# A sequence-mixing kernel on one core: the rows of a chunk are put in another order by the band, and the output goes out in runs of 8, 7 and 3 tokens

## What is computed

```python
# x: (8, 4224, 192), weight: (8 heads, 7 taps); all float32 in DRAM
w = softmax(weight)                                  # per head, over the 7 taps
y[b, s, h, :] = sum_k w[h, k] * x[b, s - 6 + k, h, :]   # causal convolution; 24 columns a head
W_tok = ((y @ w_q) @ (y @ w_k).T) / 8                # d_hyper = 64
out = relu(W_tok @ y) @ w_out                        # (8, 4224, 192)
```

## Time and profile before

| | |
|---|---|
| median of 3 runs | 185.6 us (184.69 to 186.93) |
| the profiled execution: its time, its span | 185.72 us, 184.0 us |
| DMA queue q0 (loads of x): packets, MB | 36,832, 13.96 |
| DMA queue q1 (stores, weights): packets, MB | 14,448, 26.45 |
| mean granted clock of TensorE | 0.952 of full speed |

### The profile page before, as it was taken

The page is one execution under the profiler, slowest core; times in us unless marked ns, Lnnn a source line. Parts: engine busy times, 40 slices in busy tenths (PEclk is TensorE's granted clock), DMA queues, the critical chain, the costliest instruction groups (busy, mean ns, idle before and its releaser), DMA issues.

```text
span 184.0 us, 5172 instructions
## 1 busy us (share of the span) xinstructions
PE 154.7 (84%) x2213; PEld 102.9 (56%) x2213; DVE 126.4 (69%) x207; ACT 124.5 (68%) x257; POOL 28.4 (15%) x35
## 2 busy tenths in 40 slices
PE   6876989999999999999599999892999898993500
PEld 2335745744867865667466776572755665572300
DVE  5346589786878886999668983991669979662100
ACT  2222479999686988968499759834479799894300
POOL 7910039952310600000000000000000000000000
PEclk9997899999999999999999999999699999999665
DMA  3999949999999999999999991890589699888896
GB/s 33 154 196 197 199 57 120 192 193 193 192 296 332 211 194 212 338 276 297 249 277 338 204 223 61 236 302 6 155 259 316 229 303 269 248 281 284 251 287 193
DMA packets 51302, 40.72 MB, mean 221 GB/s; under 512 B 38928, under 2 KB 44560, under 8 KB 51280
## 3 DMA queue, kind: packets, MB, share of 16 engines
q0 software_dynamic: 36832, 13.96, 64.1%
q1 hardware_dynamic: 14448, 26.45, 45.6%
HBM read 28.39 MB, written 25.95 MB: 295 GB/s over the span
## 4 chain that ended last, share of the span: by engine, by line
DMA 41%; PE 29%; ACT 10%; SPq 8%; DVE 3%; issue 2%; DVEq 0%; ACTq 0%; POOLq 0%
DMA xw<-in_x_dram 30%; PE ps L322 9%; DMA out_dram<-out_sb 8%; PE ps L923 7%; PE ps L940 6%; ACT out_sb L318 5%; SPq L978 5%; DMA wqf<-in_moe_w_q_dram 3%; PE ps L877 2%; ACT y L318 2%; PE ps L865 2%; PE ps L772 1%; SPq L969 1%; PE ps L323 1%; PE ps L690 1%
## 5 line engine op out<-in xcount | busy, mean ns | idle before, releaser
L318 ACT COPY out_sb<-ps 128x768 f32<-128x768 f32 (+2 forms) x68 | 38.9, 611 | 17.0 <-PE ps L940 10.9
L318 ACT CAST y<-ps 128x432 bf16<-128x432 f32 (+3 forms) x60 | 36.5, 650 | 12.7 <-PE ps L322 9.7
L671 DVE STREAM_TRANSPOSE yt<-y 128x864 uint32<-128x864 uint32 x32 | 33.4, 1059 | 4.6 <-ACT y L318 4.6
L895 ACT ACTIVATE rt<-ps 128x512 bf16<-128x512 f32 (+4 forms) x65 | 33.5, 559 | 2.8 <-PE ps L865 2.2
L896 DVE TENSOR_SCALAR rt<-ps 128x512 bf16<-128x512 f32 (+4 forms) x47 | 29.4, 651 | 8.1 <-PE ps L865 3.9
L500 POOL DMA_DIRECT2D xw<-in_x_dram x30 | 28.0, 948 | 34.7 <-DVE xw L511 16.4
L318 DVE COPY out_sb<-ps 128x384 f32<-128x384 f32 (+2 forms) x34 | 22.5, 684 | 15.5 <-PE ps L940 10.4
L322 PE MATMUL ps<-y 120*128 120x192 bf16 (+1 forms) x288 | 30.4, 253 | 2.7 <-ACT y L318 2.7
L940 PE MATMUL ps<-wol,rt 128*128 128x192 bf16 (+3 forms) x280 | 30.1, 258 | 0.2
L923 PE MATMUL ps<-woh,rt 64*128 64x192 bf16 (+1 forms) x280 | 26.1, 261 | 3.9 <-DVE out_sb L318 2.9
L322 PEld LDWEIGHTS ps<-y 120*128 120x128 bf16 (+1 forms) x288 | 24.7, 101 | 7.9 <-ACT y L318 3.2
(11 more groups left out here) (88 smaller groups left out, 119.5 us busy)
## 6 DMA issues: line engine op xcount, KB each, us to landing
out_dram<-out_sb SPq DMA_DIRECT2D x42, 384.0 KB, 5.5
xw<-in_x_dram POOLq DMA_DIRECT2D x7, 864.0 KB, 27.5
xw<-in_x_dram POOLq DMA_DIRECT2D x7, 672.0 KB, 30.6
out_dram<-out_sb SPq DMA_DIRECT2D x14, 288.0 KB, 5.2
out_dram<-out_sb SPq DMA_DIRECT2D x24, 96.0 KB, 3.4
out_dram<-out_sb SPq DMA_DIRECT2D x12, 192.0 KB, 2.8
xw<-in_x_dram POOLq DMA_DIRECT2D x7, 168.0 KB, 17.7
xw<-in_x_dram POOLq DMA_DIRECT2D x2, 432.0 KB, 8.2
```

What stands on the lines that cost most here:

```text
L318: return e.copy(dst, src) if op.engine == "ACT" else e.tensor_copy(dst, src)
L671: return e.transpose(YT[:, tb, ks, :].rearrange("p c d -> p (c d)"), Y[:, yb, ks, :].rearrange("p c d -> p (c d)").bitcast(U32))
L895: return e.activation(dst, src, AF.Relu)
```

## The change

Column j of the band makes row j of a chunk, so the order of the band's columns decides which token a partition holds. After the change, row 32a + 4m + i of a long chunk holds token 15m + 4a + i (m = 0 to 7; for a = 3, i = 3 the column is zero). Behind the transposes and `fin`, a partition of the output then has 15 tokens in a row for 16 chunks: 8 of them in the stretch of blocks 0 and 1, 7 in that of blocks 2 and 3. Each stretch is one DMA of 128 runs of 6,144 or 5,376 bytes. For the short chunks a second band, `BAND2`, puts token 3s + a on row 32a + s; the tail is one DMA of 128 runs of 2,304 bytes. With it:

- `BAND2` is built by two more PE operations (`spread2`) and two evacuations; the convolution of a group with short chunks takes two matmuls a head in place of one (14 chunks with `BAND`, 4 with `BAND2`);
- the short chunks load all 128 rows, so `zero_x`, `zero_xl` and the wait of the loads for them are gone; batch 1's first chunk is loaded in two pieces like batch 0's, so its `zero_c` is gone;
- block 3 is 32 columns wide in the queries, `mix` and `relu` (before 24); `fin` leaves out the zero fourth token of block 3; the tail's queries are evacuated in order, not strided;
- in the last batch only stretches 0 and 2 go out in halves, each half one DMA;
- `PLAN` is another: its convolution, evacuation and store entries stand in another order, with 107 joined evacuations (91 before). Seven store entries now stand together behind batch 3 (`586S 467S 477S 596S 544S 558S 572S`); four stood together there before (`581S 462S 539S 472S`). It ends `... 992A2 997A2 1022D 1021D 1023S 994S 999S`.

```diff
-    CW, RW, BL = 120, 96, 32
+    CW, RW, BL, RUN = 120, 96, 32, 15
-    zero_x = zero(XW[RW:128, 0, NM:, :], "zero_x")
+    zero_o = zero(OWN[:, RUN:16], "zero_o")
-    zero_xl = zero_later(XW[RW:128, 1:, NM:, :], "zero_xl")
+    zero_b = zero_later(BAND2[:, :, RW:], "zero_b")
...
-                    bank(op.bank)[:, 64 * q : 64 * q + 64].rearrange("p (i h) -> p i h", h=4),
-                    STEPT[0:112, 112 - 16 * q : 240 - 16 * q],
-                    TAPS[0:112, :, 4 * half : 4 * half + 4],
+                    bank(op.bank).rearrange("p (a m i h) -> p m a i h", a=NB, m=8, i=4)[:, q],
+                    STEPT[0:112, 112 - RUN * q : 240 - RUN * q],
+                    TAPS[0:112, :, 4 * half : 4 * half + 4].rearrange("p (a i) h -> p a i h", a=NB),
...
+        def spread2(e, op, half=half):
+            last = None
+            for q in range(7):
+                n = min(5, BL - 5 * q)
+                last = halves(
+                    e,
+                    bank(op.bank)[:, 0 : 4 * RW].rearrange("p (a s h) -> p a s h", a=3, h=4)[:, :, 5 * q : 5 * q + n, :],
+                    STEPT[0:112, 112 - RUN * q : 240 - RUN * q],
+                    TAPS[0:112, 0 : 3 * n, 4 * half : 4 * half + 4].rearrange("p (u a) h -> p a u h", a=3),
...
-                parts.append(rows(NM, NR, 0, ROWS, RW))
+                parts.append(rows(NM, NR, 0, 128, RW))
...
-                needs=([zero_xl if b else zero_x] if cs and cs[-1] == NCC - 1 and dst.shape[0] == ROWS and b < NX else []) + free,
+                needs=free,
...
+        runs = [(BAND, c0, sum(c < NM for c in cs)), (BAND2, max(c0, NM), sum(c >= NM for c in cs))]
...
+                    for band, c, m in runs:
+                        last = halves(
+                            e,
+                            PS[:, o + (c - c0) * GRP : o + (c - c0 + m) * GRP],
+                            band[:, h, :],
+                            XW[:, xb, c : c + m, GRP * h : GRP * h + GRP],
...
-        ns = (2 * TW, TW) if tail else [16 * TOKENS[a] for a in BLOCK[j]]
+        ns = (2 * TW, TW) if tail else (NQ, NQ)
...
-        pieces = 2 if b == B - 1 and not tail else 1
+        pieces = 2 if b == B - 1 and j % 2 == 0 and not tail else 1
...
-            todo = [(i, a) for i in (q, q + 1) for a in range(2) if not tail or (i, a) != (1, 1)]
+            todo = [(i, a) for i in (q, q + 1) for a in range(2) if i < has[a]]
...
                     if tail:
-                        for k in range(3):
-                            dst = bass.AP(out_t, (b * S + t0[NM] + BL * k) * D, [[D, BL], [RW * D, NR], [1, D]])
-                            sent.append((e.dma_start(dst, OUT[:, oslot, k % 2, k // 2, :]), 16))
-                        return sent
-                    for z in range(2):
-                        src = OUT[0 : rows[z], oslot, z, qa:qz, :].rearrange("p q d -> p (q d)")
-                        dst = bass.AP(
-                            out_t,
-                            (b * S + t0[16 * (j // 2)] + BL * BLOCK[j][z] + qa) * D,
-                            [[CW * D, 16], [nt * D, rows[z] // 16], [1, (qz - qa) * D]],
-                        )
-                        sent.append((e.dma_start(dst, src), 16))
-                    return sent
+                        dst = bass.AP(out_t, (b * S + t0[NM]) * D, [[3 * D, 128], [1, 3 * D]])
+                        return e.dma_start(dst, OUT[:, oslot, 0, 0:3, :].rearrange("p q d -> p (q d)"))
+                    t = b * S + t0[16 * (j // 2)] + 8 * (j % 2) + qa
+                    if pieces > 1:
+                        dst = bass.AP(out_t, t * D, [[RUN * D, 128], [4 * D, 2], [1, (qz - qa) * D]])
+                        return e.dma_start(dst, OUT[:, oslot, :, qa:qz, :].rearrange("p a q d -> p a (q d)"))
+                    m = sum(has) * D
+                    src = OUT[:, oslot, :, :, :].rearrange("p a q d -> p (a q d)")[:, 0:m]
+                    return e.dma_start(bass.AP(out_t, t * D, [[RUN * D, 128], [1, m]]), src)
```

More of the change, by code:

```diff
@@ L244, in bass_lightweight_conv__then__hypermixer_token_mlp_kernel @@
     BLOCK = ((0, 1), (2, 3), (1, 0), (3, 2))
-    TOKENS = [min(BL, CW - BL * a) for a in range(NB)]
     NSB = len(BLOCK) + 1
@@ L466, in bass_lightweight_conv__then__hypermixer_token_mlp_kernel, with band2 @@
             bands.append(add("ACT" if half == 0 else "DVE", band, cols=256, drains=fill, kind="band"))
+    bands2 = []
+    for half in range(2):
+        def spread2(e, op, half=half):
[7 more added lines that the diff above has]
+                    TAPS[0:112, 0 : 3 * n, 4 * half : 4 * half + 4].rearrange("p (u a) h -> p a u h", a=3),
+                    mode=op.mode,
+                    start=q == 0,
+                    stop=q == 6,
+                    skip_group_check=True,
+                )
+            return last
+        fill = add("PE", spread2, needs=[taps, stept], after=fills, banks=1, vt=0.05, whole=True, kind="spread2")
+        def band2(e, op, half=half, fill=fill):
+            src = bank(fill.bank)[:, 0 : 4 * RW].rearrange("p (j h) -> p h j", h=4)
+            return copy(e, op, BAND2[:, 4 * half : 4 * half + 4, 0:RW], src)
+        bands2.append(add(both, band2, cols=4 * RW, drains=fill, vt=0.05, kind="band2"))
     load = {}
@@ L858, in gen_mix @@
         nt = n // 128
-        rows = (128, 128) if tail else [m // nt for m in ns]
+        place = (0, 1) if tail else [a % 2 for a in BLOCK[j]]
+        has = (2, 1) if tail else [min(4, RUN - 4 * a) for a in BLOCK[j]]
         def mix_lo(e, op):
@@ L940, in fin_other @@
                     last = e.matmul(
-                        bank(fh.bank + a)[0 : rows[a], (i - q) * D : (i - q) * D + D],
-                        RT[p, slot, a, columns(i, a)],
+                        bank(fh.bank + place[a])[:, (i - q) * D : (i - q) * D + D],
+                        RT[p, slot, a, columns(i)],
                         WOL[p, :],
@@ L953, in gen_mix, with ev_out @@
             readers += [fh, fl]
-            def ev_out(e, op, a, z, q=q, fh=fh):
-                m = 1 if tail and a else 2
-                src = bank(fh.bank, 2).rearrange("p (t n) -> p t n", t=2)[:, a:z, 0 : m * D]
-                dst = OUT[:, oslot, a:z, q : q + m, :].rearrange("p t q d -> p t (q d)")
+            ms = [sum(place[a] == i for _, a in todo) for i in range(2)]
+            def ev_out(e, op, a, z, q=q, fh=fh, ms=ms):
+                src = bank(fh.bank, 2).rearrange("p (t n) -> p t n", t=2)[:, a:z, 0 : ms[a] * D]
+                if tail:
+                    dst = OUT[:, oslot, 0:1, a : 3 - a : 2, :]
+                    src = src.rearrange("p t (q d) -> p t q d", d=D)
+                else:
+                    dst = OUT[:, oslot, a:z, q : q + ms[a], :].rearrange("p t q d -> p t (q d)")
```

168 lines of the change are left out of this document (80 added, 88 removed).

## The result

The changed kernel takes 169.25 us (median of four runs, 168.56 to 170.49), the kernel before 185.77 beside it (184.69 to 186.93): a ratio of 0.912, 95% interval 0.904 to 0.920. The forecast was 175.2 us with a range of 168 to 185: the direction is right, the gain is 16.5 us where 10.4 were forecast. The profiled execution has a span of 168.3 us.

The account below looks back on a forecast made before the run. Transfers were taken as the bound, with DMA 41% of the chain. Span 184.0 - 2.5 (loads) + 0.5 (PE) - 2.5 - 2.5 (standstills) - 3.5 (end) = 173.5, plus 1.7 outside: 175.2 us, range 168 to 185.

Parts of the forecast that it names:

- Loads, -2.5: Loads from batch 2 on come 2.5 us earlier without the memset wait; bounds 0 and -4.1 us.
- PE, +0.5: 64 added matmuls with `BAND2` against at least 32 fewer in `fin`: net -4.7 to +3.2 us, taken as +0.5.
- ACT and DVE, 0: Wider relu of block 3, unstrided tail queries, more joins and two evacuations on ACT and DVE: 0 us together.
- slower, PE bound: Added convolution matmuls cost PE as much as existing ones, 0.225 us each: 192.2 us; chance of slower 0.11.
- Stores in the stream: Five DMAs a batch in place of eleven end the rate dips at tails; the gain goes to the two standstills.
- per byte I expect little: Store rate with packets twice as long: anything from the same 336 GB/s to another 9%.
- The two standstills, -2.5 each: Waits for an `OUT` slot before 126.52 and 168.60 us shrink by 2.5 us each; at most 3.57 and 3.98.
- The end, -3.5: From last evacuation to end of span, called issue-bound: 10.5 us becomes 7.0, bounds 4.0 and 10.5.
- loads crowded out: Longer store packets halve the loads' rate beside stores, cutting the load term to -0.6: 177.1 us; chance 0.12.
- compute sets the pace: PE, busy 38.63 of 44.1 us in the last phase, can't close up; only the end shortens: 182.2 us; chance 0.16.
- no change: Stream dips are late data, not issue, and as much stays behind the last evacuation: 184 to 187 us; chance 0.11.
- What would show it: Signs listed for loads, PE, stores and end, such as 42 issues and 326 GB/s or more, plus three signs against.

Follow-up runs that it names:

- x2_stores: Kernel before, old order, band and loads, with only the changed kernel's store DMAs (one a stretch, one a tail), tokens misplaced: 169.25 us, 0.913.
- x1_loads: Kernel before with only the short chunks loading all 128 rows, so loads wait for no memset: 182.1 us, 0.982.
- x3_both: Kernel before, old order and band, with the edits of both x1_loads and x2_stores, tokens misplaced: 167.25 us, 0.908.
- x6_hold0: Changed kernel with three stores of batch 1 made to wait for batch 4's first load: 163.41 us, 0.883 of the kernel before.
- x11_form16c: Changed kernel, each whole stretch stored as 16 pieces of 8 touching runs, same run lengths, tokens misplaced: 167.64 us, 0.912 of the kernel before.
- x12_perm: Changed kernel, same 128 places in another order over the partitions, three dimensions that can't be folded, tokens misplaced: 168.31 us, 0.912 of the kernel before.
- x13_again: Changed kernel unaltered, run again on another chip: median 169.06 us of six, five at 168.35 to 170.91 and one at 163.63.
- the two executions above: Profiled executions of the changed kernel's instructions: its own, with the standstill before batch 4 (span 168.3 us), and one of a rewritten but identical kernel, without it.

## Why the prediction was right, and where it was off

- **The number.** 169.25 us lies 1.25 above the low end of the range, and that is in part luck: without the standstill, which the sum had no term for, the same instructions take 163 to 165 us, under the range, as eight of eighteen executions did. The low end of 168 took PE's idle time from 107 to 173.5 us, 9.5 us, for all that the terms could share; the idle time ahead of it and the clock were left out.
- **Bound.** Right: the transfers set the pace, and the stores alone gave 15.5 us (x2_stores).
- **Loads, -2.5.** Right in size on the old stores (x1_loads, -2.7); on top of the new ones its worth is not clear of noise (x3_both).
- **PE, +0.5; ACT and DVE, 0.** Nothing speaks for a loss: x6_hold0 has 149.3 us of busy PE and x3_both, with the old matmuls, 149.8. In the timeline of PE after, the 96-column matmuls with `BAND2` are followed 0.04 us later by the next (both halves side by side):

```profile
57.67 0.21 PE L321 MATMUL ps<-xw,band 128*64 128x96 bf16 x1
57.67 0.21 PE L322 MATMUL ps<-xw,band 128*64 128x96 bf16 x1
57.71 0.31 PE L321 MATMUL ps<-xw,band 128*64 128x336 bf16 x1
```

  The rival "slower, PE bound" is out.
- **Stores in the stream.** The step that failed in size is "per byte I expect little", with 336 GB/s and at most 9% more. 405 GB/s at a share of 1.02 is 397 at full share, 18% above 336. The bound was drawn from the size of the packets, and of that it was right: in the old form 6,144-byte runs do no better than 3,072-byte ones did (322 to 349, x11_form16c and x12_perm). What gave the 18% is the form of the DMA, which no row of before varied and which was not thought of.
- **The two standstills, -2.5 each.** They went, but PE's idle time up to the last evacuation fell by 7.0 in x2_stores, not 5.0: PE's stop of 2.03 us before 91.72, at the end of ACT's wait for a load, shrank to 0.64 as well, though the loads had not changed. And a term was missing, the clock that PE loses behind a standstill: some 3.2 of the 5.3 us of busy time. In the changed kernel itself idle time fell by 7.0 with the new standstill (18.85 to 11.9 in x13_again) and by 12.0 without it (6.9 in x6_hold0).
- **The end, -3.5.** That issuing made the old end long was right, the size too small: 10.45 to 4.5 us, -6.0. That it comes near the bound that counted issue alone (3 x 0.64 + 2.1 = 4.0) is chance: two of the three stores were issued before the last evacuation had ended, one issue takes 0.38 us, and the rest is the way of the last data (4.1 us from issue to landing for such a half, by the page of the profile, not 2.1).
- **Rival "loads crowded out".** It happened, as a mechanism: 45 GB/s of loads became 30 (the sum had 28 and 14, both too low). But its price was put where POOL's queue is late as a whole, 1.9 us; what it cost was one load that the memset at the head of DVE's queue waited for, some 5 us (6.8 us of span between the two executions above). Forecast and rival were not alternatives: the kernel had both, a gain from the stores that was forecast too small and a standstill that was priced too low, and the two errors partly cancel.
- **Rivals "compute sets the pace" and "no change".** Out: the stream closed up by far more than the end alone. Only now, with PE at 67% of the chain, does compute set the pace.
- **What would show it.** Hole at 24 to 28, 42 issues, rate, no wait on a slot of `OUT` over 2 us, an end under 8 us: all as named. Of the signs against the forecast the last, PE's idle time coming back as waits for loads, was seen too, for one load: 5.2 us of PE at 60 to 65 us. It took back a part of the gain and not the whole.

## To carry to other kernels

Write a store so that its destination folds into 128 rows of one run, and look at what was issued, not at what was written: an access pattern of 16 x 8 rows is either the same DMA or one that is up to a fifth slower, depending on its strides. When stores get longer packets, look for the load that lands last beside them, and let the stores that start just ahead of it wait; three such waits were worth some 5 us here. Price a standstill at its length and, where one follows, at the slower clock behind it.

## What the hardware showed that was not expected

- A store with 16 outermost in three dimensions: 288 to 347 GB/s in most full windows (385 to 397 in three late ones) and 0.57 us an issue; with 128 outermost in two dimensions 405 to 412 GB/s and 0.34 us, the same bytes, the same run length.
- A standstill of PE of 5.2 us (5.7 on DVE) is followed by two windows of four microseconds at a granted clock of 0.56 and 0.59.
- Two kinds of execution, 5 us apart, from the same instructions; in the two compared the first stores start 0.8 us apart.
